# Linear attention, ELU feed-forward and dense experts on one core: the attention output written transposed by products on strips of 32 columns

## What is computed

```python
for t in range(S):
    cur = np.einsum('bhd,bhe->bhde', u[None] * kt, vt)
    y[:, :, t] = np.einsum('bhd,bhde->bhe', rt, state + cur)
    state = wt[:, :, :, None] * state + np.einsum('bhd,bhe->bhde', kt, vt)
```

## Time and profile before

| What | us |
|---|---|
| Runs: lowest, median, highest of 3 | 691.5, 695.74, 696.39 |
| The profiled execution, its own time | 691.54 |
| Its span in the trace | 689.3 |
| PE busy | 680.3 |
| DVE busy | 263.1 |
| ACT busy | 181.3 |
| POOL busy | 163.0 |

### The profile page before, as it was taken

One profiled execution on the slowest core, in us unless ns is written; L12 is line 12 of the kernel. 1 busy time (PEld: TensorE's weight loads), 2 busy tenths in 40 slices (PEclk: granted clock), 3 DMA queues, 4 the chain that ended last, 5 costly groups with the idle time before them and its releaser, 6 DMA issues.

```text
span 689.3 us, 10234 instructions
## 1 busy us (share of the span) xinstructions
PE 680.3 (99%) x3971; PEld 601.9 (87%) x3971; DVE 263.1 (38%) x471; ACT 181.3 (26%) x339; POOL 163.0 (24%) x181
## 2 busy tenths in 40 slices
PE   8999999999999999999999999999999999999998
PEld 6888999978888888899999999999999999999997
DVE  7786867666534333312121312121213121212122
ACT  3753443433335444311111111111111111111110
POOL 3899321111000466600006600016400000000000
PEclk9999999999999999999999999999999999999999
DMA  9923222220000332300003200013100000001011
GB/s 340 405 92 96 101 82 82 82 81 1 1 1 0 93 92 92 92 2 0 1 24 91 69 1 0 0 26 98 60 1 0 0 1 0 1 1 46 0 46 47
DMA packets 12854, 38.70 MB, mean 56 GB/s; under 512 B 1552, under 2 KB 3344, under 8 KB 12816
## 3 DMA queue, kind: packets, MB, share of 16 engines
q1 hardware_dynamic: 12528, 37.77, 16.1%
q10 hardware_dynamic: 288, 0.39, 0.2%
HBM read 35.80 MB, written 2.36 MB: 55 GB/s over the span
## 4 chain that ended last, share of the span: by engine, by line
PE 92%; POOL 4%; DVE 1%; issue 1%; ACT 1%; DMA 0%; DVEq 0%; POOLq 0%
PE bank L878 29%; PE bank L880 28%; PE bank L879 28%; POOL w_lo L376 3%; PE bank L831 3%; PE bank L784 1%; PE bank L821 1%; PE bank L808 1%; PE bank L795 1%; PE bank L842 1%; DMA rkw<-rkw_dram 0%; POOL tok L357 0%; DVE fr L527 0%; DVE w_lo L613 0%; POOL tok L360 0%
## 5 line engine op out<-in xcount | busy, mean ns | idle before, releaser
L878 PE MATMUL bank<-x_lo,w_hi 128*128 128x512 f32 (+2 forms) x480 | 181.7, 378 | 2.5 <-POOL w_lo L376 2.2
L726 DVE SCALAR_TENSOR_TENSOR g_lo<-bank,g_hi 128x512 fp32r<-128x512 f32 x96 | 66.4, 692 | 308.4 <-ACT g_hi L495 308.4
L880 PE MATMUL bank<-x_hi,w_hi 128*128 128x512 f32 (+2 forms) x480 | 178.7, 372 | 0.0
L879 PE MATMUL bank<-x_hi,w_lo 128*128 128x512 f32 (+2 forms) x480 | 177.4, 370 | 0.0
L495 ACT ACTIVATE g_hi<-bank 128x512 fp32r<-128x512 f32 x96 | 57.5, 599 | 341.0 <-PE bank L880 341.0
L880 PE MATMUL bank<-w_hi,g_hi 128*128 128x384 f32 x384 | 129.7, 338 | 0.0
L879 PE MATMUL bank<-w_hi,g_lo 128*128 128x384 f32 x384 | 129.6, 337 | 0.0
L878 PE MATMUL bank<-w_lo,g_hi 128*128 128x384 f32 x384 | 129.3, 337 | 0.0
L880 PEld LDWEIGHTS bank<-x_hi,w_hi 128*128 128x128 f32 x480 | 90.1, 188 | 17.5
L878 PEld LDWEIGHTS bank<-x_lo,w_hi 128*128 128x128 f32 x480 | 90.2, 188 | 16.0 <-issue 3.0
L879 PEld LDWEIGHTS bank<-x_hi,w_lo 128*128 128x128 f32 x480 | 90.4, 188 | 12.7
(11 more groups left out here) (67 smaller groups left out, 559.9 us busy)
## 6 DMA issues: line engine op xcount, KB each, us to landing
raw<-w_dram SPq DMA_DIRECT2D x48, 384.0 KB, 3.1
rkw<-rkw_dram SPq DMA_DIRECT2D x10, 772.5 KB, 4.4
tok<-tok_dram SPq DMA_DIRECT2D x12, 576.0 KB, 4.4
out_dram<-acc SPq DMA_DIRECT2D x10, 192.0 KB, 1.9
rkw<-rkw_dram SPq DMA_DIRECT2D x2, 512.0 KB, 4.6
rkw<-rkw_dram SPq DMA_DIRECT2D x2, 260.5 KB, 3.6
out_dram<-acc ACTq DMA_DIRECT2D x2, 192.0 KB, 2.0
u_rep<-u_dram SPq DMA_DIRECT2D x1, 192.0 KB, 6.6
```

What stands on the lines that cost most here:

```text
L726: dve.scalar_tensor_tensor(out=g2[1][:, r, :], in0=p_h[j % 2][:, :], scalar=0.0, in1=g2[0][:, r, :].bitcast(F32), op0=ALU.max, op1=ALU.sub ...
L878: pe.matmul(out, wh, ml, start=start, stop=False)
L879: pe.matmul(out, wl, mh, start=False, stop=False)
L880: return pe.matmul(out, wh, mh, start=False, stop=stop)
```

## The change

The output of attention is made transposed, in PSUM, in one place. `yt` is now written in strips of 32 of its 384 rows (12 strips, four on the partitions of one 128-column block), with tokens along the free dimension. The stationary operand is a strip of 32 columns of the state or of v, the moving operand is r or `att` with 128 columns. The state `st` is block-diagonal for a pair of heads (128 rows by 96 columns, with zeros where the heads do not meet), so that one product serves both heads. A strip in the middle of a pair holds 16 columns of each head: the even head's half is a product of 16 columns, and the odd head's half comes from `v_odd`, a copy of 16 columns of v beside 16 of zeros, which ACT makes for each chunk (`copy_odd`). The bonus is turned by products with the identity (`turn_bonus`). `finish_y` and `turn_y` are gone, and `hi_x` reads `yt` when the products are done. `old_values` stands behind `down1` now, next to `values`.

The place in time changes too. Scores come one step later (`SCORES`, 4c for 4c-1). `hi_x` and `lo_x` come at s+3, which is the same step n as before. DVE takes slices 8 and 10 of `w_lo` and `bonus_v(1)` from POOL. `add_update` is two operations on 64 partitions, and `scale_state` covers 384 columns for 192. Here is the diff, cut to its core:

```diff
-SCORES = {c: 4 * c - 1 for c in range(FIRST, NC)}
+SCORES = {c: 4 * c for c in range(FIRST, NC)}
...
-LO_VECTOR = (0, 3, 5)
-LO_POOL = (1, 2, 4, 6, 7, 8, 9, 10, 11, 12, 13, 14, 15)
-LO_BETWEEN = {1: ((5, 0),)}
-LO_AFTER = {0: ((3, 0), (3, 1)), 2: ((5, 1),)}
+LO_VECTOR = (0, 3, 5, 8, 10)
+LO_POOL = (1, 2, 4, 6, 7, 9, 11, 12, 13, 14, 15)
+LO_BETWEEN = {1: (5, 0), 3: (8, 0), 5: (10, 0), 6: (10, 1)}
+LO_AFTER = {0: ((3, 0), (3, 1)), 2: ((5, 1),), 4: ((8, 1),)}
+STRIP = 32
+STRIPS = DM // STRIP
...
-            st = sb("st", [P, 2, PAIRS, D], scope=scope)
-            y_sb = sb("y_sb", [P, 2, DM], scope=scope)
+            st = sb("st", [P, 2, PAIRS, PD], scope=scope)
+            bonus_v_sb = sb("bonus_v_sb", [P, 2, DM], scope=scope)
+            v_odd = sb("v_odd", [P, 2, PAIRS, STRIP], scope=scope)
...
             def load_tok(c):
                 need(sp, s_py, c - DEEP + 1)
                 need(sp, s_pu, min(c - DEEP + 1, NUPDATE))
                 need(sp, s_cv, c - DEEP + 1)
+                need(sp, s_odd, c - DEEP + 1)
...
+            def copy_odd(c):
+                landed(act, s_tok, c)
+                need(act, s_py, c - 1)
+                if c == 0:
+                    act.wait_ge(s_zero, 4)
+                odd = v_of(c).rearrange("p (a e) -> p a e", a=PAIRS)[:, :, D:D + STRIP // 2]
+                act.copy(v_odd[:, c % 2, :, STRIP // 2:STRIP], odd).then_inc(s_odd, 1)
...
                 for c in due(n, 1):
                     if c < NUPDATE:
                         copy_kt(c, BESIDE)
+                    copy_odd(c)
...
-                dve.tensor_tensor(st[:, c % 2, :, :], banks["u"].rearrange("p (a e) -> p a e", a=PAIRS),
-                                  st[:, c % 2, :, :], ALU.add).then_inc(s_sum, 1)
+                for o in range(2):
+                    rows = slice(64 * o, 64 * o + 64)
+                    own = st[rows, c % 2, :, o * D:(o + 1) * D]
+                    dve.tensor_tensor(own, banks["u"][rows, :].rearrange("p (a e) -> p a e", a=PAIRS), own,
+                                      ALU.add).then_inc(s_sum, 1)
...
-            def finish_y(c, banks):
-                dve.wait_ge(s_cv, c + 1)
-                dve.wait_ge(s_py, c + 1)
-                y = y_sb[:, c % 2, :].rearrange("p (a o e) -> p o a e", o=2, e=D)
-                for o in range(2):
-                    dve.tensor_tensor(y[:, o], banks["y"][o].rearrange("p (a e) -> p a e", e=D), y[:, o],
-                                      ALU.add).then_inc(s_y, 1)
...
+            dve.wait_ge(s_cv, 1)
+            bonus_v(1)
             lo_w(0, 0)
-            finish_y(0, BANKS0)
-            finish_y(1, BANKS1)
             lo_w(0, 1)
...
+            def turn_bonus(c, yt, first):
+
+                pe.wait_ge(s_cv, c + 1)
+                if first:
+                    pe.wait_ge(s_kt, min(c + 1, NUPDATE))
+                    pe.wait_ge(s_x, c)
+                for k in range(KT):
+                    ins = pe.matmul(yt[:, k * P:(k + 1) * P], bonus_v_sb[:, c % 2, k * P:(k + 1) * P], ident,
+                                    start=first and k == 0, stop=True, skip_group_check=True)
+                if not first:
+                    ins.then_inc(s_py, 1)
+
+            def old_values(c, yt):
+
                 pe.wait_ge(s_st, c - 1)
                 q = q_of(c)
...
+                for b in range(STRIPS):
+                    p, first = b // 3, b % 3 * STRIP
+                    pe.matmul(strip_of(yt, b), st[:, c % 2, p, first:first + STRIP], q[:, p * CH:(p + 1) * CH],
+                              start=False, stop=True, skip_group_check=True)
+
+            def values(c, yt):
 
                 landed(pe, s_tok, c)
                 pe.wait_ge(s_att, c * 2 + 2)
+                pe.wait_ge(s_odd, c + 1)
                 v = v_of(c)
...
+                for b in range(STRIPS):
+                    p, first = b // 3, b * STRIP
+                    columns = STRIP // 2 if b % 3 == 1 else STRIP
+                    pe.matmul(strip_of(yt, b)[0:columns], v[:, first:first + columns], att[:, b % 3 // 2, p, :],
+                              start=False, stop=True, skip_group_check=True)
+                for p in range(PAIRS):
+                    ins = pe.matmul(strip_of(yt, 3 * p + 1), v_odd[:, c % 2, p, :], att[:, 1, p, :],
+                                    start=False, stop=True, skip_group_check=True)
+                ins.then_inc(s_val if c < FIRST else s_py, 1)
...
-            fill(4, 1)
-            values(0, BANKS0)
-            fill(2, 1)
+            fill(3, 1)
+            fill(1, 2)
+            values(0, BANKS0["yt"])
+            fill(5, 1)
...
-            fill(1, 2)
-            values(1, BANKS1)
-            turn_y(0, BANKS0)
-            turn_y(1, BANKS1)
-            fill(4, 1)
+            fill(1, 4)
+            values(1, BANKS1["yt"])
+            turn_bonus(0, BANKS0["yt"], False)
+            turn_bonus(1, BANKS1["yt"], False)
+            fill(3, 3)
...
                 for c in due(n, 2):
-                    old_values(c, BESIDE)
+                    turn_bonus(c, BESIDE["yt"], True)
                 if n >= LAG:
                     down1(n - LAG)
...
                 for c in due(n, 2):
-                    values(c, BESIDE)
+                    old_values(c, BESIDE["yt"])
+                    values(c, BESIDE["yt"])
                 for c in due(n, 3):
                     if c < NUPDATE:
                         update(c, BESIDE)
-                    turn_y(c, BESIDE)
```

More of the change, by code:

```diff
@@ L397, in _ @@
             bonus_v(0)
-            bonus_v(1)
             lo_w(1)
@@ L440, in _ @@
             copy_kt(0, BANKS0)
+            copy_odd(0)
             hi_w(0)
             hi_w(1)
+            copy_odd(1)
             hi_w(2)
@@ L446, in _ @@
             hi_w(4)
-            hi_w(5)
             hi_x(0, BANKS0["yt"])
             hi_x(1, BANKS1["yt"])
-            for n in range(6, HI_FIRST):
+            for n in range(5, HI_FIRST):
                 hi_w(n)
@@ L475, in _ @@
             for n in range(STEP1):
-                for c in due(n, 4):
+                for c in due(n, 3):
                     hi_x(c, BESIDE["yt"])
@@ L682, in _ @@
                 for c in due(n, 3):
-                    finish_y(c, BESIDE)
+                    lo_x(c, BESIDE["yt"])
                 for c in due(n, 4):
@@ L696, in _ @@
                     add_update(1, BANKS1)
-                for part in LO_BETWEEN.get(n, ()):
-                    lo_w(*part)
-                if n == SCALE_K[FIRST]:
+                if n in LO_BETWEEN:
+                    lo_w(*LO_BETWEEN[n])
+                if n == INVERSES[FIRST] + 1:
                     alphas(FIRST)
@@ L811, in update, with strip_of @@
                 ins.then_inc(s_pu, 1)
-            def old_values(c, banks):
-                pe.wait_ge(s_att, c * 2 + 2)
+            def strip_of(yt, b):
+                rows = slice(b % 4 * STRIP, b % 4 * STRIP + STRIP)
+                return yt[rows, b // 4 * P:b // 4 * P + P]
+            def turn_bonus(c, yt, first):
[8 more added lines that the diff above has]
+                    ins.then_inc(s_py, 1)
@@ L816, in old_values @@
+            def old_values(c, yt):
                 pe.wait_ge(s_st, c - 1)
                 q = q_of(c)
-                for h in range(H):
-                    p, o = h // 2, h % 2
-                    rows = slice(64 * o, 64 * o + D)
-                    pe.matmul(banks["y"][o][:, p * D:(p + 1) * D], q[rows, p * CH:(p + 1) * CH],
-                              st[rows, c % 2, p, :], start=h < 2, stop=False, skip_group_check=True)
-            def values(c, banks):
+                for b in range(STRIPS):
+                    p, first = b // 3, b % 3 * STRIP
+                    pe.matmul(strip_of(yt, b), st[:, c % 2, p, first:first + STRIP], q[:, p * CH:(p + 1) * CH],
+                              start=False, stop=True, skip_group_check=True)
@@ L826, in values @@
+            def values(c, yt):
                 landed(pe, s_tok, c)
                 pe.wait_ge(s_att, c * 2 + 2)
+                pe.wait_ge(s_odd, c + 1)
                 v = v_of(c)
-                for h in range(H):
-                    p, o = h // 2, h % 2
-                    ins = pe.matmul(banks["y"][o][:, p * D:(p + 1) * D], att[:, o, p, :],
-                                    v[:, h * D:(h + 1) * D], start=c < FIRST and h == 0, stop=True,
-                                    skip_group_check=True)
```

67 lines of the change are left out of this document (31 added, 36 removed).

## The result

| | before | after |
|---|---|---|
| median, us (lowest to highest) | 693.63 (691.48 to 696.39), 6 runs | 683.97 (683.71 to 684.42), 6 runs |
| profiled execution, us | 691.54 | 684.12 |
| its span, us | 689.3 | 682.3 |
| first product of up(48), the first step behind all attention products | 212.29 | 204.58 |

What follows compares the result with a forecast made beforehand. PE was taken as the bound beside the feed-forward steps; -6.7 - 2.7 - 0.3 + 0.3 = -9.4 us gave 682.1 from the profiled execution, 686.3 from the median; 685.5 was predicted, range 679 to 701.

Steps and rivals of the forecast that it cites:

- four strips at once: Forecast case for the attention strip products: four run at once, 0.028 us a pass; chance 0.60.
- What bounds the kernel: From 60 to 90 us PE is busy 29.95 of 30.00; taking an instruction from PE shortens the run, from DVE not.
- Attention, -6.7: PE's attention products: a chunk costs 2.62 us instead of 3.29; ten chunks beside the feed-forward steps give -6.7 us.
- The rule that spoke against it: Skill's strict program order for matmuls: next strip's first pass joins only the second, so two at once, 0.056 a pass.
- two at once: Rival for the strip products: two run at once, 0.056 us a pass, +6.5 us, 702.2; chance 0.12.
- The waits for `w_lo`, -2.7: PE's three waits for POOL's w_lo in the first sixteen steps all go, since POOL loses slices 8 and 10: -2.7 us.
- The loop of ACT and DVE until step 8: In steps 3 to 8 this loop, more than PE, sets the pace, g_hi 2.34 us apart, and it stays.
- DVE's extra work, +0.3: DVE's w_lo halves and second additions, 3.6 us in steps 0 to 6, mostly hidden: +0.3; from chunk 2 on even.
- Moved waits, "nothing": turn_bonus's wait for kt_sb ahead of down1 costs nothing, up to 0.3 us a chunk if ACT slips.
- Prologue, -0.3: Before step 0: it starts near 19.6, 0.6 us earlier; the ACT and DVE loop eats part, leaving -0.3.
- 733: Rival for the strip products: one at a time, 0.112 us a pass, +4.0 us a chunk, 733; chance 0.05.
- DVE becomes the bound: Rival for steps 1 to 8: DVE's 3 us of added work come in full, 688.7 to 689; chance 0.12.

Runs made afterwards that it cites:

- experiment 3: Changed kernel with turn_bonus made as a transpose, one pass per block instead of two, for chunks 2 to 11: 681.86 us, ratio 0.9849.
- experiment 1: Changed kernel with all strips on one part of the array: 732.42 us; with three neighbouring strips sharing a part: 694.29; with strips alternating between two parts: 685.47.
- experiment 2's first kernel: Changed kernel with slices 8 and 10 of w_lo given back from DVE to POOL: 686.8 us, ratio 0.9932.

## Why the prediction was right

The forecast, four strips at once, came true, with 683.97 for 685.5 in a range of 679 to 701. Its steps one by one:

- **What bounds the kernel: right.** An instruction taken from PE shortened the run (experiment 3), if not where DVE runs behind it.
- **Attention, -6.7: right in mechanism, a little too small.** It is -7.6. The 0.028 a pass is 0.027 (0.109/4), entry and exit are 0.34 for 0.38, `turn_bonus` is 0.67 as said. That makes 2.54 a chunk where 2.62 was predicted, and ten times this 0.08 is the miss, but for 0.1.
- **The rule that spoke against it.** "TensorE: Matmul & The Clock Gate", section "Part 3: Packing small matmuls — row/col tiling", of the Trainium skill, has matmuls start and end in strict program order. The measurement decides against it here: in experiment 1 matmuls of later products start ahead of those of earlier ones (79.21 ahead of 79.28 to 79.53). Fours start together in the changed kernel, so two at once, and with it 702.2, did not come. The same section's 2.38 times for three column tiles, scaled to four, made the estimate of 3.2 times and 0.035 a pass. Here the price of a pass on four strips is 0.027 against 0.106 on one, 3.9 times less.
- **The waits for `w_lo`, -2.7: right,** all three went (2.8 by the starts); the slices alone are worth 2.3 at up(48) in the changed kernel. That they also bite through DVE was not seen. The sign that went with it, up(13) some 3.5 us earlier, came at 2.0 (58.56 to 56.55), as the new waits for `g_lo` and at `scores` lie ahead of it.
- **The loop of ACT and DVE until step 8: right, and its consequence missed.** `g_hi` stands 2.34 apart still (35.74, 38.08). But `scores` of chunk 2, 1.6 us of PE's work at step 7, had covered DVE's lateness; moved to step 8 it leaves up(8) waiting 1.0 us for `g_lo`. With the other waits of these steps it is +1.3, of which 0.3 stands before `down1`: new idle for `g_lo` was one of the prediction's own signs of being wrong, and it came. That the moved `scores` are the cause is read from the traces; no run has them at step 7 in the changed kernel.
- **DVE's extra work, +0.3: right for the halves, in itself.** Against experiment 2's first kernel they cost 0.3 at up(6) and 0.2 at up(8). In the kernel before they cost 1.4 in waits for `g_lo`. From chunk 2 on, the other new work of DVE was taken as even by DVE's average idle time (7 us in 30), and that is where the step failed.
- **Moved waits, "nothing": wrong, +1.8.** I looked at the two waits of `turn_bonus` (both cost nothing) and not at `scores`, whose waits for DVE the diff shows, too. PE came 0.8 us sooner in each chunk to a DVE that is in one piece from ELU to `add_update`, whose scaling (L572) takes 1.1 us there, and on which the change had put 0.9 us more (`bonus` 0.54, the second addition 0.38). DVE was 77% busy in that stretch, 23.09 of 30 us, and this average hid a burst.
- **Prologue, -0.3: near in size, wrong in its working.** Step 0 starts 0.02 earlier in the two traces compared, but the start of `values(1)` varies by 0.7 us between runs with the same prologue; from there on the prologue is 0.25 shorter. The working took PE's end of `turn_bonus` and added `x_hi` and `x_lo` to it, and left out that DVE had `bonus_v(1)` and slice 0 in front of `x_lo` (2.6 us from 16.56). It had step 0 at 19.6, 0.6 earlier, and then took half of that.

The misses partly cancel: -0.9 for the attention, -0.1 for `w_lo`, +1.0 for `g_lo`, +1.8 for `scores`, +0.3 for the start of step 0 in these two traces, -0.5 for two small waits, +0.7 for the last stores, -0.4 around the span (1.8 us for 2.2): +1.9 on a sum of -9.4, where own times differ by 7.4. The forecast itself lay 3.4 above the sum's 682.1 for the sake of the median's group near 696, which has no counterpart in the changed kernel; so that it came out only 1.5 too high is the luck of two opposite errors. The rivals' times of 702.2 and 733 were counted from that median, too; from the profiled execution they would be 698 and 729. Of the rivals, "DVE becomes the bound" had a part of the truth: 1.3 us in steps 3 to 8, though hardly by the halves, and 1.8 at the `scores` of steps 12 to 28, which it did not name.

## What to carry to other kernels

When the bounding engine's work shrinks at one place of a repeating pattern, follow it to the next instruction that waits for another engine, and ask whether that engine is in one piece just before; its mean busy share does not show this. When a piece of work is moved, ask which wait it was hiding where it stood. And products that use a part of the array pay when they are spread over all its parts: here that was worth a factor of four for a pass, and 48 us. The order matters less, since PE goes past one waiting product: three neighbours on the same part cost 10 us, two parts in turn 1.5.

## What the runs showed of the hardware that was not expected

- PE starts a later product ahead of an earlier one whose part of the array is busy (a matmul at 79.21 ahead of those at 79.28 to 79.53), past one waiting product for a part, so a poor order of the strips costs less than strict order would: 10 us for triples and 1.5 for two parts in turn, where 39 and 13 were expected.
- The same DVE operation takes very different times beside POOL: the half of a `w_lo` slice 0.55 us or 0.99 at the same place of the program in two runs, the scaling (L572) 0.68 or 1.13 us. In the changed kernel's trace it depends on who is first. At 67.37 POOL's operation had 0.58 us left, and the scaling took 1.13; the same at 81.50, 95.15, 108.80 and 122.44. At 142.24 POOL's had 0.10 left and its next began 0.06 later: the scaling took 0.68, as with POOL idle, and POOL's next 1.08 where it mostly takes 0.60. A table of mean durations hides this, and a wait of 0.3 us can come or go with it.
- A transpose of a float32 block costs one pass, 0.11 us, and the strips added onto what it left in PSUM as they did onto a product with the identity.
